# Fused product with its rounded parts first, a re-ordered start, two sums of a double tile started later, and the last output and its stores in another order

## The chip, the cores and the metric

The kernel runs on one core of one Trainium2 chip. The metric is the time of one execution in device microseconds, lower is better. A core has five engines that run side by side, each with its own instruction stream: PE (matrix products, into the eight banks of PSUM), DVE (elementwise work of vectors), ACT (activations and copies), POOL (a further, slower elementwise engine) and SP, which here only issues transfers. They wait for each other by semaphores.

## The reference

Three layers follow each other on 4608 tokens (8 batches of 576) with 512 features. All data are fp32.

```python
def _attn_ref(q, k, v, p):                 # 8 batches, 8 heads, 576 x 64; p: 32 packed rows
    p_packed = sm_attn(p, k, v)
    return sm_attn(q, p_packed, p_packed)

def _moe_ref(x, w_gate, w_val, w_out, rms_g):       # 512 -> 1536 -> 512
    rms = np.sqrt(np.mean(x * x, axis=-1, keepdims=True) + 1e-06)
    xn = x / rms * rms_g
    g = xn @ w_gate
    silu = g * (1.0 / (1.0 + np.exp(-g)))
    return silu * (xn @ w_val) @ w_out

def _moe2_ref(x, w1, w2, w3, w_out):                # 512 -> 1024 -> 1024 -> 512
    h = (x @ w1) * (x @ w2) @ w3
    return h @ w_out
```

## The kernel before

**Three products for one.** PE multiplies fp32 numbers quickly in a rounded format. Every operand is split into a rounded part `hi` (a copy on ACT) and the rest `lo` (a subtraction on DVE that needs `hi`); a product is `hi·hi + hi·lo + lo·hi`, three matmuls added in PSUM. A matmul of 512 columns starts about 0.227 us behind the one in front of it.

**Stage 1, the start.** Since nothing stands between `w3` and the last `w_out`, their product `wf` (1024 x 512) is formed once. `fuse(half, c, rows)` on PE does chunk c of 8 for half of `wf`: four blocks (`rows`) of three matmuls each. Before it, SP loads the chunk (`load_fuse`), ACT rounds (`fuse_split`), DVE subtracts. Into this work the attention of batch 0 is woven by hand, as *items*: S1 (scores), AT (transposes), PV, PT, G, S2, Z, SS (sum of squares), M (gate and value weights folded with the packed values, six pieces). An item has its PE part and behind it parts on ACT and DVE; two items that use the same banks need the older one's parts done (`xy_free`). The order of the calls is written out once for each engine, and `FIRST_ITEMS` numbers the items. From SS comes the reciprocal root of the mean square: `ms` on DVE, `eps` added and the power taken on POOL (`inverse_rms`), a store and a broadcast load through memory (`spread_r`), POOL scales `a2T` with it (`scale_a2`), ACT and DVE split it (`a2_split`); the loop needs that.

**Stage 2, the loop.** 192 slots n (`into` and `outof` on PE) go over the gated layer of all batches; the next batch's items lie between them (`SLOT_ITEMS`). Gate and value have one bank each, so `into(n)` waits until DVE has read slot n-1 (`u_ready`, `h_ready`). `wo_split` splits the output weights in slots of the first batch.

**Stage 3, the last layer.** A tile of 256 columns (t = 0) and four *double tiles* of 512 go through four pairs p each; g counts the 20 groups. A group has seven products in a Strassen-like scheme, P1, P6, P7, P4, P5, P2, P3, which DVE adds up (`e1`, `u2`, `u3`, `c21`, ...) into `h` (four quarters, each a product of two sums), which is split again and goes through `outof2` or `outof_wide` with `wf`. The first double tile starts at g = 4. Its operands are sums of quarters of x that POOL makes in `sum_x(t)`: `b12`, `t2`, then `t4` (for P4) and `t1` (for P5); ACT and DVE split each. Between P6 and P7 of g = 4 PE does `outof2(3)`; P7 then needs the banks that DVE empties in `evict2`.

**The end.** The last group's `outof_wide` (16 blocks of three matmuls: 8 column blocks m, each for f = 1 and f = 0) is followed by DVE's `add_out(m)` and a store of block m.

## Time and profile before

| what | value |
|---|---|
| time of three runs | median 1333.63 us (1332.37 to 1334.44) |
| the profiled execution: own time, span of its instructions | 1333.3 us, 1331.5 us |
| PE busy | 1314.6 us, 99% of the span, 8592 matmuls |
| DVE, ACT, POOL busy | 875.4, 411.1, 125.2 us |
| PE's granted clock, mean | 0.998 of full speed |

The span goes from the first to the last instruction; the execution's own time lies 1.8 us above it. A matmul's end is modelled and overlaps the next one's start, so PE counts as busy up to 0.16 us after it could have started the next; a share of 99% leaves room for short waits that the busy time does not show. They are seen in the starts: where two matmuls of 512 columns lie further apart than 0.227 us, PE stood.

### The profile page before, as it was taken

Reading aid. Unit: us, or ns where it says so; the run is one execution under the profiler, and the core shown is the slowest. Engines: PE = TensorE matmul, PEld = TensorE weight load, DVE = VectorE, ACT = ScalarE, POOL = GpSimd, SP = SyncE. Lnnn points to the kernel's source line nnn. Section 1 sums busy time; section 2 is a strip of 40 time slices with the busy share of each in tenths; the row PEclk is TensorE's granted clock in tenths of the full one; section 3 lists DMA queues with packets and bytes.
Section 4 is the critical chain, followed back from the end, with each engine's and each line's share of the span. In section 5 each row is a group of like instructions: output and inputs, shape, how many; then the busy total and the mean of one; then the engine's idle time right before and its main releaser. Section 6 shows DMA issues by size and latency. Waiting matters only on the chain.

```text
span 1331.5 us, 21676 instructions
## 1 busy us (share of the span) xinstructions
PE 1314.6 (99%) x8592; PEld 1090.7 (82%) x8592; DVE 875.4 (66%) x1363; ACT 411.1 (31%) x785; POOL 125.2 (9%) x101
## 2 busy tenths in 40 slices
PE   8999999999999999999999999899999999999998
PEld 6788888888878788887889899788888888888886
DVE  4668657576565765756754667766776686677665
ACT  5344433434434344343333433210200120112000
POOL 0200101001000010010100531100200010020000
PEclk9999999999999999999999999999999999999999
DMA  9683434343534435333326486745454335545202
GB/s 352 223 282 124 156 124 154 126 163 109 176 97 162 160 117 162 122 118 105 113 74 231 184 313 261 245 136 182 141 175 158 127 119 197 175 144 192 91 1 64
DMA packets 117203, 211.41 MB, mean 159 GB/s; under 512 B 33904, under 2 KB 35952, under 8 KB 114032
## 3 DMA queue, kind: packets, MB, share of 16 engines
q1 hardware_dynamic: 90992, 203.73, 44.8%
q10 hardware_dynamic: 26112, 6.30, 2.1%
q8 instruction: 69, 1.13, 0.4%
q14 instruction: 30, 0.25, 0.1%
HBM read 168.04 MB, written 41.96 MB: 158 GB/s over the span
## 4 chain that ended last, share of the span: by engine, by line
PE 96%; DVE 2%; DMA 1%; issue 1%; ACT 0%; SPq 0%; DVEq 0%; ACTq 0%
PE psum L946 9%; PE psum L948 8%; PE psum L947 8%; PE psum L834 8%; PE psum L836 8%; PE psum L835 8%; PE psum L860 7%; PE psum L859 7%; PE psum L858 7%; PE psum L988 4%; PE psum L990 4%; PE psum L989 4%; PE psum L793 3%; PE psum L777 1%; PE psum L874 1%; PE psum L872 1%
## 5 line engine op out<-in xcount | busy, mean ns | idle before, releaser
L834 PE MATMUL psum<-a_hi,m_hi 128*128 128x288 f32 x768 | 235.5, 307 | 1.9 <-DVE g_s L1529 1.0
L836 PE MATMUL psum<-a_hi,m_lo 128*128 128x288 f32 x768 | 226.3, 295 | 0.0
L835 PE MATMUL psum<-a_lo,m_hi 128*128 128x288 f32 x768 | 226.3, 295 | 0.0
L834 PEld LDWEIGHTS psum<-a_hi,m_hi 128*128 128x128 f32 x768 | 144.2, 188 | 47.5 <-issue 39.3
L1529 DVE SCALAR_TENSOR_TENSOR g_s<-g_s,psum 128x288 f32<-128x288 f32 x192 | 86.7, 452 | 129.6 <-ACT g_s L1243 128.7
L860 PE MATMUL psum<-g_hx,wo_lo 128*128 128x512 f32 x384 | 152.1, 396 | 0.0
L859 PE MATMUL psum<-g_hx,wo_hi 128*128 128x512 f32 x384 | 151.4, 394 | 0.0
L1248 ACT CAST g_hx<-g_h 128x288 fp32r<-128x288 f32 x192 | 83.1, 433 | 219.5 <-DVE g_h L1535 214.5
L858 PE MATMUL psum<-g_hx,wo_hi 128*128 128x512 f32 x384 | 150.2, 391 | 0.0
L835 PEld LDWEIGHTS psum<-a_lo,m_hi 128*128 128x128 f32 x768 | 144.4, 188 | 5.1
L836 PEld LDWEIGHTS psum<-a_hi,m_lo 128*128 128x128 f32 x768 | 144.1, 188 | 0.0
L1547 DVE TENSOR_TENSOR g_hx<-g_h,g_hx 128x288 fp32r<-128x288 f32 x192 | 90.4, 471 | 70.1 <-ACT g_hx L1248 70.1
L1307 ACT CAST hhd<-hd_raw 128x1024 fp32r<-128x1024 f32 x16 | 16.9, 1054 | 317.7 <-DVE hd_raw L1633 309.0
L1243 ACT ACTIVATE g_s<-psum 128x288 f32<-128x288 f32 x192 | 78.9, 411 | 91.3 <-PE psum L836 89.9
L988 PE MATMUL psum<-wf_hi,hhd 128*128 128x512 f32 x256 | 100.4, 392 | 0.1
L990 PE MATMUL psum<-wf_hi,hd_lo 128*128 128x512 f32 x256 | 99.7, 389 | 0.0
L989 PE MATMUL psum<-wf_lo,hhd 128*128 128x512 f32 x256 | 99.7, 389 | 0.0
L946 PE MATMUL psum<-xd_hi,w_hi 128*128 128x512 f32 x224 | 88.0, 393 | 4.7 <-DVE u L1654 4.7
L1476 DVE TENSOR_TENSOR bd<-bd,psum 128x512 f32<-128x512 f32 x96 | 65.9, 687 | 40.6 <-PE psum L990 39.5
L1535 DVE SCALAR_TENSOR_TENSOR g_h<-g_s,psum 128x288 f32<-128x288 f32 x192 | 87.1, 454 | 6.9 <-DVE g_s L1529 0.3
L947 PE MATMUL psum<-xd_lo,w_hi 128*128 128x512 f32 x224 | 87.8, 392 | 0.0
L948 PE MATMUL psum<-xd_hi,w_lo 128*128 128x512 f32 x224 | 87.6, 391 | 0.0
(188 smaller groups left out, 2437.6 us busy)
## 6 DMA issues: line engine op xcount, KB each, us to landing
w_in<-in_w_gate SPq DMA_DIRECT2D x24, 1024.0 KB, 7.3
w_in<-in_w_val SPq DMA_DIRECT2D x24, 1024.0 KB, 5.2
wb_hi<-w_scratch SPq DMA_DIRECT2D x56, 256.0 KB, 2.8
wb_lo<-w_scratch SPq DMA_DIRECT2D x56, 256.0 KB, 3.1
w_hi<-w_scratch SPq DMA_DIRECT2D x49, 256.0 KB, 2.9
w_lo<-w_scratch SPq DMA_DIRECT2D x49, 256.0 KB, 3.7
kT<-in_kT SPq DMA_DIRECT2D x8, 1152.0 KB, 7.5
v_sb<-in_v SPq DMA_DIRECT2D x8, 1152.0 KB, 10.1
```

Source lines behind the costliest of these rows:

```text
L834: nc.tensor.matmul(in_ps[which], hi, a2_hi[:, t, par, :], start=par == 0, stop=False)
L835: nc.tensor.matmul(in_ps[which], hi, a2_lo[:, t, par, :], start=False, stop=False)
L836: last = nc.tensor.matmul(in_ps[which], lo, a2_hi[:, t, par, :], start=False, stop=par == 1)
L858: nc.tensor.matmul(out_ps[m], hi, hh, start=f == 0, stop=False)
L859: nc.tensor.matmul(out_ps[m], hi, hl, start=False, stop=False)
L860: last = nc.tensor.matmul(out_ps[m], lo, hh, start=False, stop=f == FC - 1)
L946: nc.tensor.matmul(dst, hi, xhi[:, c, :], start=c == 0, stop=False)
L947: nc.tensor.matmul(dst, hi, xlo[:, c, :], start=False, stop=False)
L948: last = nc.tensor.matmul(dst, lo, xhi[:, c, :], start=False, stop=c == 1)
L988: nc.tensor.matmul(dst, hhd[:, f, cols], wf_hi[:, chunk, :], start=f == 1, stop=False)
L989: nc.tensor.matmul(dst, hhd[:, f, cols], wf_lo[:, chunk, :], start=False, stop=False)
L990: last = nc.tensor.matmul(dst, hld[:, f, cols], wf_hi[:, chunk, :], start=False, stop=f == 0)
```

## The change

Six things, in the order of the program:

1. `fuse` issues the four `hi·hi` matmuls of a chunk first, then the four `hi·lo`, then the four `lo·hi`, and waits for each part only there; the last chunk keeps the order of before, block by block. Seven warming matmuls are issued and not eight.
2. The third chunk is loaded ahead of `kT`. The order of items and chunks is written anew on PE, ACT and DVE; the two rounding steps (`exp1(1, 0)`, `a2_split`) of the loop's first needs stand ahead of `wf_evict(1)`. The item M(0, 2) moves from the start into slot 0 of the loop, its DVE part to the end of slot 1, and `wo_split(0)` into slot 1.
3. `eps` is added on DVE and no longer on POOL; `spread_r(0)` is issued ahead of `load_w_in(0, 2)`.
4. For the first double tile POOL starts `t4` and `t1` only when the fourth group's last quarter of `h` is there (`h12_ready`), and DVE makes `lo` of the first half of `h` ahead of the `lo` of P6's operand.
5. In the last `outof_wide`, f = 0 of block m follows f = 1 of block m+3 (`LEAD`), where all of f = 1 came first.
6. The last two column groups of x change places, so that the blocks m = 0..3 hold the batches' remainders; of each of their two stores one is issued by SP and one by ACT.

```diff
-FIRST_ITEMS = [..., ("Z", 0, 0), ("Z", 0, 1), ("M", 0, 0), ("SS", 0, 0), ("S1", 1, 0), ("M", 0, 1), ("S1", 1, 1), ("M", 0, 2)]
+FIRST_ITEMS = [..., ("Z", 0, 0), ("Z", 0, 1), ("SS", 0, 0), ("M", 0, 0), ("S1", 1, 0), ("M", 0, 1), ("S1", 1, 1)]
-WARM = 8
+WARM = 7
 # SP
-            load_fuse(0, 0)
-            load_fuse(0, 1)
+            for c in range(3):
+                load_fuse(0, c)
             load_kp(0)
...
             store_wf(0)
+            spread_r(0)
             load_w_in(0, 2)
-            spread_r(0)
...
-                    sp.dma_start(out_batches[B - 1, P * m:P * (m + 1), :], bd[:, m, :]).then_inc(out_stored, 16)
+                    sp.dma_start(out_batches[2 * m, TILE2:S, :], bd[0:REST, m, :]).then_inc(out_stored, 16)
                 else:
-                    for h in range(2):
-                        sp.dma_start(out_batches[2 * (m - 4) + h, TILE2:S, :], bd[REST * h:REST * (h + 1), m, :]).then_inc(out_stored, 16)
+                    sp.dma_start(out_batches[B - 1, P * (m - 4):P * (m - 3), :], bd[:, m, :]).then_inc(out_stored, 16)
 # POOL
                 pool.wait_ge(x_sum_ready, 4 * t + 2)
+                if t == 1:
+
+                    pool.wait_ge(h12_ready, PAIRS)
 # PE, fuse
+                for group in ([(m,) for m in rows] if last_chunk else [rows]):
+                    for m in group:
...
+                        nc.tensor.matmul(psum[:, fuse_bank[r], :], w3_hi[half][:, c, P * m:P * (m + 1)], wout_hi[:, c, :],
+                                         start=c == 0, stop=False)
+                    if half == 0 and not last_chunk:
+                        pe.wait_ge(wout_lo_ready, c + 1)
...
+                    if not last_chunk:
+                        pe.wait_ge(w3_lo_ready, FC2 * half + c + 1)
 # PE, the end
-            for f in (1, 0):
-                for m in range(BLOCKS2):
-                    if f == 1:
-                        block_free(GROUPS - 1, m)
-                    outof_wide(GROUPS - 1, m, f)
+            for m in range(BLOCKS2 + LEAD):
+                if m < BLOCKS2:
+                    block_free(GROUPS - 1, m)
+                    outof_wide(GROUPS - 1, m, 1)
+                if m >= LEAD:
+                    outof_wide(GROUPS - 1, m - LEAD, 0)
 # ACT, the end
+            for m in range(4):
+                act.wait_ge(bd_ready, BLOCKS2 * (PAIRS * WIDE - 1) + m + 1)
+                nc.scalar.dma_start(out_batches[2 * m + 1, TILE2:S, :], bd[REST:P, m, :]).then_inc(out_stored, 16)
 # DVE
+                    nc.vector.tensor_scalar(ms[:], ms[:], EPS_RMS, None, ALU.add).then_inc(ms_ready, 1)
...
+                if g < GROUPS - 1:
+                    rest2(1)
                 for u in late[2]:
                     unit(u)
-                if g < GROUPS - 1:
-                    rest2(1)
```

**The first chunk on PE.** Rows of PE's order behind the warming matmuls, first of the kernel before (the lines 809, 810, 811 are the three products of a block):

```order
L996 MATMUL psum<-ident 128x128 x8
L809 MATMUL psum<-wout_hi,w3a_hi 128x512
L810 MATMUL psum<-wout_lo,w3a_hi 128x512
L811 MATMUL psum<-wout_hi,w3a_lo 128x512
L809 MATMUL psum<-wout_hi,w3a_hi 128x512
L810 MATMUL psum<-wout_lo,w3a_hi 128x512
L811 MATMUL psum<-wout_hi,w3a_lo 128x512
```

and of the changed kernel, where a row with x4 stands for the four blocks:

```order
L1015 MATMUL psum<-ident 128x128 x7
L819 MATMUL psum<-wout_hi,w3a_hi 128x512 x4
L824 MATMUL psum<-wout_lo,w3a_hi 128x512 x4
L829 MATMUL psum<-wout_hi,w3a_lo 128x512 x4
L819 MATMUL psum<-wout_hi,w3a_hi 128x512 x4
L824 MATMUL psum<-wout_lo,w3a_hi 128x512 x4
L829 MATMUL psum<-wout_hi,w3a_lo 128x512 x4
L819 MATMUL psum<-wout_hi,w3a_hi 128x512 x4
L824 MATMUL psum<-wout_lo,w3a_hi 128x512 x4
L829 MATMUL psum<-wout_hi,w3a_lo 128x512 x4
L737 MATMUL psum<-kT,pT 32x288 x16
```

The part that needs only the two rounded operands now stands four matmuls ahead of the first that needs `wout_lo`, and eight ahead of the first that needs `w3a_lo`; three chunks stand ahead of the first item (S1, L737).

**The step to the double tile.** DVE's order of the fourth group's end and of the first double tile, before (`h_lo` is the rest of a half of `h`, `xd_lo` that of an operand of the double tile):

```order
L1640 TENSOR_TENSOR e<-e,psum 128x512
L1647 TENSOR_TENSOR h_raw<-e 128x256
L1451 TENSOR_TENSOR xd_lo<-t,xd_hi 128x1024
L1574 TENSOR_TENSOR h_lo<-h_raw,hh 128x512
L1654 TENSOR_TENSOR u<-u,psum 128x512
L1656 TENSOR_TENSOR h_raw<-u 128x256
L1574 TENSOR_TENSOR h_lo<-h_raw,hh 128x512
L1451 TENSOR_TENSOR xd_lo<-xd_raw,xd_hi 128x1024
L1586 TENSOR_TENSOR u2d<-e1d,psum 128x1024
```

and changed:

```order
L1670 TENSOR_TENSOR e<-e,psum 128x512
L1677 TENSOR_TENSOR h_raw<-e 128x256
L1604 TENSOR_TENSOR h_lo<-h_raw,hh 128x512
L1476 TENSOR_TENSOR xd_lo<-t,xd_hi 128x1024
L1684 TENSOR_TENSOR u<-u,psum 128x512
L1686 TENSOR_TENSOR h_raw<-u 128x256
L1604 TENSOR_TENSOR h_lo<-h_raw,hh 128x512
L1476 TENSOR_TENSOR xd_lo<-xd_raw,xd_hi 128x1024
L1616 TENSOR_TENSOR u2d<-e1d,psum 128x1024
```

The `lo` of the first half of `h` has moved ahead of that of P6's operand (`xd_lo<-t`). POOL's rows with their waits there, before and changed:

```order
L692 TENSOR_TENSOR t<-x 128x1024 [waits b11_loaded,x_sum_ready]
L698 TENSOR_TENSOR xd_raw<-x,t 128x1024 [waits prod_done6,b21_loaded,x_sum_ready]
L701 TENSOR_TENSOR xd_raw<-x,t 128x1024 [waits prod_done4]
```

```order
L694 TENSOR_TENSOR t<-x 128x1024 [waits b11_loaded,x_sum_ready]
L703 TENSOR_TENSOR xd_raw<-x,t 128x1024 [waits b21_loaded,prod_done6,h12_ready,x_sum_ready]
L706 TENSOR_TENSOR xd_raw<-x,t 128x1024 [waits prod_done4]
```

The third sum, and the fourth behind it, now wait for `h12_ready`, which DVE gives with the last `h_raw<-u` of the group.

**The end.** PE's order with its waits from block m = 3 on (`hl2_ready0` stands for f = 0), in the changed kernel, where the kernel before had the twelve matmuls of f = 1 for the blocks 4 to 7 in their place:

```order
L1007 MATMUL psum<-wf_hi,hhd 128x512 [waits hl2_ready1,u4_ready]
L1008 MATMUL psum<-wf_lo,hhd 128x512
L1009 MATMUL psum<-wf_hi,hd_lo 128x512
L1007 MATMUL psum<-wf_hi,hhd 128x512 [waits hl2_ready0]
L1008 MATMUL psum<-wf_lo,hhd 128x512
L1009 MATMUL psum<-wf_hi,hd_lo 128x512
L1007 MATMUL psum<-wf_hi,hhd 128x512 [waits hl2_ready1,c11_ready]
L1008 MATMUL psum<-wf_lo,hhd 128x512
L1009 MATMUL psum<-wf_hi,hd_lo 128x512
```

The first block that needs `hl2_ready0` is now the fifth of sixteen and not the ninth. The last stores on SP before:

```order
L614 DMA out<-bd 128x512 [waits bd_ready] x4
L617 DMA out<-bd 64x512 [waits bd_ready]
L617 DMA out<-bd 64x512
L617 DMA out<-bd 64x512 [waits bd_ready]
L617 DMA out<-bd 64x512
```

and changed:

```order
L620 DMA out<-bd 64x512 [waits bd_ready] x4
L622 DMA out<-bd 128x512 [waits bd_ready] x4
L140 UNCONDITIONAL_BRANCH [waits out_stored]
```

SP has eight to issue in the place of twelve, and its last one covers 128 rows; four of 64 rows are issued by ACT.

## Rows read from the trace of the kernel before

**Rows 1.** The page, part 1: busy time, share of the span, count.

```profile
PE 1314.6 (99%) x8592; PEld 1090.7 (82%) x8592; DVE 875.4 (66%) x1363; ACT 411.1 (31%) x785; POOL 125.2 (9%) x101
```

**Rows 2.** The waits of PE, longest first in total: us, times, longest.

```profile
PE psum L946 <- DVE u L1654: 4.7, 1, 4.7
```

**Rows 3.** Timeline of the start: us from the start, duration, what, idle before.

```profile
4.42 0.62 ACT L1126 CAST w3a_hi<-w3a_raw 128x512 fp32r<-128x512 f32 x1 [0.39 <-DMA w3a_raw<-in_w3T]
5.82 0.50 PE L809 MATMUL psum<-wout_hi,w3a_hi 128*128 128x512 f32 x1 [0.79 <-DVE w3a_lo L1409]
```

**Rows 4.** Timeline around the third chunk of the fused product.

```profile
12.66 0.69 DVE L1409 TENSOR_TENSOR w3a_lo<-w3a_raw,w3a_hi 128x512 fp32r<-128x512 f32 x1
...
13.41 0.50 PE L809 MATMUL psum<-wout_hi,w3a_hi 128*128 128x512 f32 x1 [0.65 <-DVE w3a_lo L1409]
```

**Rows 5.** Timeline of PE: three later waits in the fused product.

```profile
32.52 0.50 PE L809 MATMUL psum<-wout_hi,w3a_hi 128*128 128x512 f32 x1 [0.39 <-DVE w3a_lo L1409]
...
35.87 0.50 PE L809 MATMUL psum<-wout_hi,w3b_hi 128*128 128x512 f32 x1 [0.34 <-DVE w3b_lo L1409]
...
42.89 0.50 PE L809 MATMUL psum<-wout_hi,w3b_hi 128*128 128x512 f32 x1 [0.25 <-DVE w3b_lo L1409]
```

**Rows 6.** Timeline of POOL: the reciprocal root of batch 0.

```profile
50.66 1.18 POOL L649 TENSOR_TENSOR ms<-ms,eps_rms 96x6 f32<-96x6 f32 x1 [3.46 <-DVE ms L1337]
51.91 1.34 POOL L653 TENSOR_TENSOR rr<-ms,neg_half 96x6 f32<-96x6 f32 x1
```

**Rows 7.** Timeline of DVE: the rounding rest of batch 0's first half.

```profile
62.05 1.27 DVE L1400 TENSOR_TENSOR a_lo<-a2T,a_hi 128x576 fp32r<-128x576 f32 x1 [0.91 <-ACT a_hi L1119]
```

**Rows 8.** Timeline of PE: slots 1 and 2 of the loop.

```profile
67.78 0.37 PE L834 MATMUL psum<-a_hi,m_hi 128*128 128x288 f32 x1 [0.32 <-DVE g_s L1529]
...
70.28 0.40 PE L834 MATMUL psum<-a_hi,m_hi 128*128 128x288 f32 x1 [0.67 <-DVE g_s L1529]
```

**Rows 9.** Timeline of DVE at the first double tile.

```profile
834.61 2.71 DVE L1451 TENSOR_TENSOR xd_lo<-t,xd_hi 128x1024 fp32r<-128x1024 f32 x1 [0.63 <-ACT xd_hi L1174]
837.24 2.83 DVE L1574 TENSOR_TENSOR h_lo<-h_raw,hh 128x512 fp32r<-128x512 f32 x1
839.99 0.68 DVE L1654 TENSOR_TENSOR u<-u,psum 128x512 f32<-128x512 f32 x1
840.70 0.42 DVE L1656 TENSOR_TENSOR h_raw<-u 128x256 f32<-128x256 f32 x1
...
845.43 1.22 DVE L1586 TENSOR_TENSOR u2d<-e1d,psum 128x1024 f32<-128x1024 f32 x1 [0.48 <-PE psum L948]
...
848.90 1.30 DVE L1458 COPY b_res<-psum 128x512 f32<-128x512 f32 x2 [1.12 <-PE psum L966]
```

**Rows 10.** Timeline of POOL at the first double tile: its two last sums.

```profile
833.56 2.68 POOL L698 TENSOR_TENSOR xd_raw<-x,t 128x1024 f32<-128x1024 f32 x1 [4.56 <-PE psum L948]
836.20 3.32 POOL L701 TENSOR_TENSOR xd_raw<-x,t 128x1024 f32<-128x1024 f32 x1
```

**Rows 11.** Windows there: length, busy by engine, PEclk, DMA share, GB/s.

```profile
836.00:840.80 4.80, 0.13 (x1) 0.02 (x1) 4.77 (x4) 0.00 (x0) 3.52 (x2) 1.00 0.97 318
840.81:844.30 3.49, 3.49 (x8) 2.77 (x9) 1.58 (x3) 3.09 (x4) 0.00 (x0) 0.51 1.04 387
```

**Rows 12.** Timeline of the end: PE, DVE, SP.

```profile
1314.27 0.47 PE L988 MATMUL psum<-wf_hi,hhd 128*128 128x512 f32 x1
...
1317.75 1.23 DVE L1574 TENSOR_TENSOR hd_lo<-hd_raw,hhd 128x1024 fp32r<-128x1024 f32 x1 [1.17 <-ACT hhd L1310]
...
1324.14 5.19 SPq L617 DMA_DIRECT2D out<-bd  x8
```

**Rows 13.** DMA issues: count, KB each, median us to landing.

```profile
r_sb<-r_scratch SPq DMA_DIRECT2D x8, 288.0 KB, 5.0
out<-bd SPq DMA_DIRECT2D x4, 256.0 KB, 2.0
out<-bd SPq DMA_DIRECT2D x8, 128.0 KB, 2.4
```

More of the change, by code:

```diff
@@ L485, in load_x @@
                 loaded = x_loaded if h else (b11_loaded, b21_loaded)[k]
-                sp.dma_start(part, x_halves[2 * t - 1 + h, k]).then_inc(loaded, 16)
+                sp.dma_start(part, x_halves[half_tile(t, h), k]).then_inc(loaded, 16)
             def load_wo(i):
@@ L490, in load_wo @@
                 sp.dma_start(wo_raw[:, rows, :], wo_v[:, rows, :]).then_inc(wo_loaded[i], 16)
-            load_fuse(0, 0)
-            load_fuse(0, 1)
+            for c in range(3):
+                load_fuse(0, c)
             load_kp(0)
-            for c in range(2, 5):
+            for c in range(3, 5):
                 load_fuse(0, c)
@@ L646, in inverse_rms @@
             def inverse_rms(a):
[L647 to L649 removed]
+                pool.wait_ge(neg_ready, 1)
                 pool.wait_ge(ms_ready, a + 1)
@@ L797, in fuse @@
             def fuse(half, c, rows=(0, 1, 2, 3)):
-                pe.wait_ge(w3_lo_ready, FC2 * half + c + 1)
+                last_chunk = c == FC2 - 1
+                pe.wait_ge(w3_hi_ready, FC2 * half + c + 1)
                 if half == 0:
-                    pe.wait_ge(wout_lo_ready, c + 1)
-                for m in rows:
-                    r = 4 * half + m
-                    if c == 0 and r >= 6:
-                        pe.wait_ge(wf_act, r - 5)
-                    cols = slice(P * m, P * (m + 1))
-                    hi, lo, dst = w3_hi[half][:, c, cols], w3_lo[half][:, c, cols], psum[:, fuse_bank[r], :]
-                    nc.tensor.matmul(dst, hi, wout_hi[:, c, :], start=c == 0, stop=False)
-                    nc.tensor.matmul(dst, hi, wout_lo[:, c, :], start=False, stop=False)
-                    last = nc.tensor.matmul(dst, lo, wout_hi[:, c, :], start=False, stop=c == FC2 - 1)
-                    if c == FC2 - 1:
-                        last.then_inc(fuse_done, 1)
+                    pe.wait_ge(wout_hi_ready, c + 1)
@@ new lines, in fuse @@
+                if last_chunk:
+                    pe.wait_ge(w3_lo_ready, FC2 * half + c + 1)
+                    if half == 0:
+                        pe.wait_ge(wout_lo_ready, c + 1)
+                for group in ([(m,) for m in rows] if last_chunk else [rows]):
+                    for m in group:
+                        r = 4 * half + m
+                        if c == 0 and r >= 6:
+                            pe.wait_ge(wf_act, r - 5)
+                        nc.tensor.matmul(psum[:, fuse_bank[r], :], w3_hi[half][:, c, P * m:P * (m + 1)], wout_hi[:, c, :],
+                                         start=c == 0, stop=False)
+                    if half == 0 and not last_chunk:
+                        pe.wait_ge(wout_lo_ready, c + 1)
+                    for m in group:
+                        nc.tensor.matmul(psum[:, fuse_bank[4 * half + m], :], w3_hi[half][:, c, P * m:P * (m + 1)], wout_lo[:, c, :],
+                                         start=False, stop=False)
+                    if not last_chunk:
+                        pe.wait_ge(w3_lo_ready, FC2 * half + c + 1)
+                    for m in group:
+                        last = nc.tensor.matmul(psum[:, fuse_bank[4 * half + m], :], w3_lo[half][:, c, P * m:P * (m + 1)], wout_hi[:, c, :],
+                                                start=False, stop=last_chunk)
+                        if last_chunk:
+                            last.then_inc(fuse_done, 1)
@@ L1235, in _ @@
                     item(*it)
-                if b + 1 < B and s in EXP1:
+                if b + 1 < B and s in EXP1 and n:
                     exp1(b + 1, EXP1.index(s))
@@ L1248, in _ @@
                 nc.scalar.copy(g_hx[f % 2][:, 0, HALF * t:HALF * (t + 1)], g_h[:]).then_inc(hh_ready, 1)
-                if n < SLOTS and t == 0:
+                if 0 < n < SLOTS and t == 0:
                     wo_split(f)
@@ L1481, in _ @@
                 nc.vector.memset(mask[NP * c:NP * (c + 1), NP * c:NP * (c + 1)], 1.0).then_inc(mask_ready, 1)
-            for c in range(3):
+            for c in range(4):
                 fuse_split(0, c)
             shift1(0)
-            fuse_split(0, 3)
+            fuse_split(0, 4)
             sums1(0)
-            fuse_split(0, 4)
-            fuse_split(0, 5)
-            fuse_split(0, 6)
+            for c in range(5, 8):
+                fuse_split(0, c)
+            freed(dve, "G", 0, 0)
             item("S2", 0, 0)
             shift2(0, 0)
+            fuse_split(1, 0)
             inner(0)
-            fuse_split(0, 7)
             sums2(0, 0)
             normalize2(0, 0)
-            fuse_split(1, 0)
             item("S2", 0, 1)
@@ L1548, in _ @@
                                         ALU.subtract).then_inc(hl_ready, 1)
-                if n < SLOTS and t == 0:
+                if n == 1:
+                    item("M", 0, 2)
+                if 0 < n < SLOTS and t == 0:
                     wo_split(f)
```

82 lines of the change are left out of this document (42 added, 40 removed).

## Prediction

> **What bounds the kernel now.** I read the page first: PE is busy for 1314.6 of 1331.5 us [rows 1], and the change takes no matmul away but one that warms. So only time in which PE stands can be won, and what of the end lies behind PE. The waits of PE come next: one is 4.7 us long, at the first double tile, the others are below a microsecond [rows 2]. Then the timelines, at three places.
>
> *The start.* PE begins the fused product at 5.82, when `w3a_lo` is there; the rounded operand was ready at 4.42 + 0.62 = 5.04 [rows 3]. It stands again before the third chunk, with 0.65 us idle shown, whose operands land behind `kT` [rows 4], and three times later with 0.39, 0.34 and 0.25 shown, each for a DVE subtraction [rows 5]. The idle time shown is not the whole loss. A matmul lasts 0.39 in the trace and the next starts 0.227 later, so 0.16 belongs on top; and where a chunk is cut in the middle, its restart (0.50 for 0.39) is 0.11 more.
>
> *The step to the double tile.* PE is through with P1 at 836.0 and P6 starts at 840.8 [rows 11]; it waits for DVE's sum `u` (839.99) [rows 2, 9]. DVE stands before it in two subtractions that take 2.71 and 2.83 us [rows 9], though the same forms take 1.22 (1024 wide; 845.43 shows that length for another add) and under 0.7 alone. POOL's `t4` (833.56, 2.68) and `t1` (836.20, 3.32) run at the same time [rows 10]. The times fit turns: DVE's first subtraction ends 1.08 behind POOL's first sum (837.32 against 836.24), the second 0.55 behind POOL's second (840.07 against 839.52). Alone a POOL sum takes about 2.3: 3.32 less the 1.1 in which DVE finished. The wait has a second price: behind it PE is granted 0.51 of its clock for 3.4 us [rows 11], so P6's twelve matmuls take 4.4 and not 2.8, 1.6 more.
>
> *The end.* SP spends 5.19 us issuing the last eight stores, from 1324.14 to 1329.33, about 0.6 each [rows 12], while the last block is summed by 1326.15. The last store lands 2.3 behind its issue at 1328.74, at 1331.1. Stores of 256 KB land 2.0 behind theirs [rows 13].
>
> **The change, part by part.**
>
> *Start.* What goes: 5.82 to 5.1 is 0.7; 0.65 + 0.16 = 0.8 before the third chunk, which is now loaded 1.25 MB earlier; 0.39 + 0.16 = 0.55; 0.34 + 0.27 = 0.6; 0.25 + 0.27 = 0.5; and three waits too short for the view, estimated at 0.2 each. Together 3.8. I followed the new order engine by engine with the durations of the trace: PE meets each `hi` and each `lo` ready, by 0.1 us at the second chunk, and by 0.4 to 2 later. The tight place is SS, which needs both `wsum` pieces: it comes out within 0.1 of PE's arrival. M(0, 2) costs its 1.2 in slot 0 and not in the start, so nothing. In slots 1 and 2 PE waited for `u` (0.32 and 0.67 shown, 1.3 with the overlap) [rows 8]. M(0, 2) covers the first; but ACT now makes `m_hi` (1.0) ahead of slot 1's tanh, and DVE `m_lo` (1.2) ahead of slot 2's sums, so about 0.9 and 0.3 stay: 0.1 gained. The eighth warming matmul is hidden either way: its time lies before 5.0. The chain to slot 0: POOL's `eps` add, 1.18 us, becomes a DVE operation of 0.2 [rows 6], and SS stands ahead of M(0, 0). Before, the rest of `a2` was ready at 62.05 + 1.27 = 63.3 [rows 7] and slot 0 began at 65.7 (67.78 less twelve matmuls of 0.13 and the 0.47 waited). Now SS is about 3 earlier and the chain 1.0 shorter: 59.2, with slot 0 at 65.7 - 3.8 - 1.3 = 60.6. It holds if `r_sb` lands in its 5.0 [rows 13], with 1.4 to spare. The `ms` add in the other seven batches lies beside PE's slots. I take 3.8 less 0.1 for SS: **3.7**. Bounds: 2.7 (two chunks late by the size of the waits seen, 0.5) and 4.6 (slot waits gone too).
>
> *The first double tile.* Without POOL beside it DVE does: `h_lo` at 833.9 to 834.6, `lo` of P6 834.6 to 835.8, `u` (0.68) to 836.5, `h` (0.42) to 836.9. PE starts P6 at 836.6 where it was 840.8, and with its clock up. POOL starts `t4` at 836.95 and ends at 839.3; DVE's next `h_lo`, ready at 837.6, gets its turn then and ends at 839.9; POOL's `t1` ends at 842.2. ACT has rounded `t4` by 840.4, but DVE's `lo` of P4 gets through only behind POOL: 842.2 + 1.1 = 843.3. Then `u2d` (1.22) to 844.5, `lo` of P5 to 845.6, and `evict2` (two copies, 1.30) [rows 9] to 846.9. P7 waits for `evict2`. PE has done P6 and `outof2(3)` at 836.6 + 2.8 + 5.4 = 844.8 and stands 2.1. Before, P7 started at 850.7 (24 matmuls behind 845.2), with `evict2` done at 850.2. So P7 comes 3.8 earlier, 0.1 of it lost in the restart: **3.7**. What is late next is thus P7. Bounds: 5.9 if POOL and DVE don't take turns there, and 2.3 if POOL's sums take 3.32 each and DVE is pushed back accordingly.
>
> The Trainium skill has the turn-taking too (GPSIMD Engine Reference, Key points: the two share their SBUF interfaces, with contention where DVE has two SBUF inputs). By that rule `u2d` and the copies, which read PSUM, run free, as I have put them; if it held for them too, `t1` would still be over by then, and the sum stays.
>
> *The end.* In the last group f = 1 of the first four blocks runs from 1314.27 for 12 x 0.227 + 0.1, to 1317.1. The fifth block-part now is f = 0 of block 0, and it needs DVE's `hd_lo`, ready at 1317.75 + 1.23 = 1318.98 [rows 12]; before, PE had work until 1319.8. So PE stands from 1317.1 to 1319.1 and ends 2.1 later: a loss of 2.1. Then DVE's last sum ends at 1328.3, SP issues one store at once, which lands after 2.0: 1330.35 where it was 1331.08. The stores gain 2.8, together **0.7**. Bounds: 2.8 if PE did not wait, and a loss of 2.1 if the stores gain nothing.
>
> The Trainium skill speaks against a gain from sharing the issues (DMA: Bandwidth & Descriptors, Issuing engines are not separate DMA queues: a second issuer saves only the issuing time, usually small beside the transfer). By it the end would lose 2.1 and the time be 1328.0; the row decides otherwise, since eight issues took 5.19 us and the last sum was over 2.6 before the last issue began.
>
> *Sum.* 3.7 + 3.7 + 0.7 = 8.1. The profiled execution took 1333.3 (span 1331.5 and 1.8 around it), 0.3 below the median of the runs: **1325.2 us**.
>
> **The rivals.**
>
> *P7 does not wait.* If POOL's sums and DVE's subtractions overlap, the middle gives 5.9: 1323.0. For it: the sums are only 2.4 long in themselves. Against it: both long subtractions end behind a POOL sum [rows 9, 10]. 12%.
>
> *The clock falls in a new gap.* After 4.7 us without a matmul it fell to 1.2 GHz and cost 1.6 [rows 11]; after the 0.67 in slot 2 it stayed up. The new gaps (2.1 at P7, 2.0 at the end) lie between. One fall gives 1326.8, two 1328.4. [...] 12%.
>
> *The start gives half.* Six places of the new order have under 0.5 us to spare; if four cost 0.5 each, the start gives 1.7: 1327.2. 11%.
>
> *The change moves the waits only.* Start 1, middle 0.7 (P7 late and the clock down), end 0: 1331.6, no change to tell. 5%.
>
> *Slower.* Slot 0 waits for the scaled `a2`. `r_sb` now has the 1 MB of `w_in(0, 2)` right behind it in the same queue, and at 51 us `w_in(0, 3)`. If it landed 9.5 us later than its 5.0, slot 0 would start past 69 and all 8.1 be gone; beyond that the kernel is slower, at 12 later 1335.8. Against it: in the trace of before a transfer of 1 MB was issued 0.4 behind it too, and it landed in 5.1. 4%.
>
> **How the numbers follow.** The forecast, with each of the three terms near its size (1323.8 to 1326.8), has 56%. Its point is the prediction. The range takes in P7 without a wait at its lower end and one or two falls of the clock or a half start at its upper end: 1321.9 to 1328.4, with some 12% left out. A measurement here tells 0.2%, 2.7 us, from no change. Faster by more holds in all cases but the last two and a part of the half start with a fallen clock: 0.91; same 0.05; slower 0.04.
>
> **What the changed profile would show.** Right: the first fused matmul at 5.1; the third chunk follows the second with no gap; slot 0 starts at 60 to 61.5; P6 of the first double tile waits about 0.6, and P7 about 2, for `evict2`; DVE's `lo` of P4 is over 2 us long; PE's clock is at 2.4 GHz there; in the last group one wait of about 1.9 for `hd_lo`; the last store lands 2.0 behind its issue. Wrong: a wait for `a2`'s rest before slot 0, for `wsum` before SS, or new waits at P4 and P5.

## The result, and the profile after

| what | before | changed |
|---|---|---|
| median, lowest, highest of five runs each (us) | 1333.55, 1332.37, 1334.44 | 1325.23, 1323.90, 1327.67 |
| ratio of the times, 95% interval | | 0.9941 [0.9926, 0.9955] |
| the profiled execution: own time, span | 1333.3, 1331.5 | 1326.28, 1324.7 |

The change makes the kernel 0.59% faster by the ratio, 8.3 us by the medians; the forecast was 1325.2. The agreement to 0.03 us is luck: the two profiled executions lie 7.0 apart and not the 8.1 of the forecast's sum, and the changed kernel's five runs spread over 3.8 us. One execution of `whole_stores_lead3`, below, took 1451.83 us at a mean granted clock of 0.847, where its other three took 1340.65 to 1342.94; it is left out of every figure. The page after the change, part 1:

```profile
PE 1313.4 (99%) x8590; PEld 1090.2 (82%) x8590; DVE 874.1 (66%) x1371; ACT 410.9 (31%) x785; POOL 121.6 (9%) x92
```

PE's busy time fell by 1.2 us against [rows 1]; the other 5.6 of the 6.8 us of span are time in which PE stood. The waits of PE now:

```profile
PE psum L965 <- DVE b_res L1483: 1.9, 1, 1.9
PE psum L1007 <- DVE hd_lo L1604: 1.8, 1, 1.8
...
PE psum L853 <- DVE g_s L1553: 0.8, 2, 0.4
PE psum L965 <- DVE u L1684: 0.5, 1, 0.5
PE psum L819 <- ACT w3a_hi L1144: 0.4, 1, 0.4
```

The 4.7 of [rows 2] has become 0.5 (`u`, ahead of P6), and two waits of nearly 2 us are new: `b_res` is `evict2`, ahead of P7, and `hd_lo` is the fifth block-part of the last group. Where the time went can be followed by the starts of the same matmul in both traces:

| the same matmul | before | changed | difference | forecast |
|---|---|---|---|---|
| first of the fused product | 5.82 | 5.37 | -0.45 | -0.7 |
| first of slot 0 | 65.72 | 62.68 | -3.04 | -5.1 (M(0, 2) now lies in the slot) |
| first of slot 4 | 76.70 | 74.61 | -2.09 | -3.7 |
| first of stage 3's double tiles (P1, g = 4) | 833.22 | 830.66 | -2.56 | -3.7 |
| first of P7, g = 4 | 850.67 | 844.36 | -6.31 | -7.4 |
| first of the last group's `outof_wide` | 1314.27 | 1308.00 | -6.26 | -7.4 |
| last matmul | 1325.04 | 1320.83 | -4.21 | -5.3 |
| last landing | 1331.08 | 1324.11 | -6.97 | -8.1 |

*Start.* Timeline of PE at the first chunk and at slot 2, changed kernel:

```profile
5.37 2.07 PE L819 MATMUL psum<-wout_hi,w3a_hi 128*128 128x512 f32 x4 [0.45 <-ACT w3a_hi L1144]
7.24 1.12 PE L824 MATMUL psum<-wout_lo,w3a_hi 128*128 128x512 f32 x3
...
67.67 0.40 PE L853 MATMUL psum<-a_hi,m_hi 128*128 128x288 f32 x1 [0.43 <-DVE g_s L1553]
```

PE now starts with ACT's rounded operand, and no wait for a subtraction is left in the fused product. But the matmuls of the first chunk stand 0.427 apart from 5.96 to 7.67, where all others stand 0.227 apart: PE runs at the lower of its two clocks, 1.2 GHz, though the page's PEclk says full speed there. That it is the clock is read from the step: where a trace does grant 0.50, as in warm8 below, the same matmuls stand 0.427 apart too. Six steps take 2.60 us (5.37 to 7.97) and not 1.47, so 1.1 us is lost. In the trace of before the first chunk runs at full speed. So the rule that PE stood wherever two such starts lie more than 0.227 us apart holds only at full clock.

*First double tile.* Timelines of DVE and POOL, changed kernel:

```profile
832.05 1.23 DVE L1476 TENSOR_TENSOR xd_lo<-t,xd_hi 128x1024 fp32r<-128x1024 f32 x1
833.19 0.68 DVE L1684 TENSOR_TENSOR u<-u,psum 128x512 f32<-128x512 f32 x1
...
835.07 2.34 DVE L1604 TENSOR_TENSOR h_lo<-h_raw,hh 128x512 fp32r<-128x512 f32 x1 [0.74 <-ACT hh L1300]
838.06 2.69 DVE L1476 TENSOR_TENSOR xd_lo<-xd_raw,xd_hi 128x1024 fp32r<-128x1024 f32 x1 [0.65 <-ACT xd_hi L1192]
840.67 1.21 DVE L1616 TENSOR_TENSOR u2d<-e1d,psum 128x1024 f32<-128x1024 f32 x1
841.80 1.21 DVE L1476 TENSOR_TENSOR xd_lo<-xd_raw,xd_hi 128x1024 fp32r<-128x1024 f32 x1
842.94 1.28 DVE L1483 COPY b_res<-psum 128x512 f32<-128x512 f32 x2
...
834.46 2.40 POOL L703 TENSOR_TENSOR xd_raw<-x,t 128x1024 f32<-128x1024 f32 x1 [8.14 <-DVE h_raw L1686]
836.82 2.85 POOL L706 TENSOR_TENSOR xd_raw<-x,t 128x1024 f32<-128x1024 f32 x1
```

The `lo` of P6's operand takes 1.23 without POOL beside it (2.71 in [rows 9]), and `u` starts 6.8 us earlier, 2.6 of them from the start. The collision has not gone but moved: the next `h_lo` (2.34) and the `lo` of P4 (2.69) now lie beside POOL's sums, and end 0.55 and 1.08 behind them, to the hundredth as before. It is the same in the traces of before, of the changed kernel and of eleven of the experiments: a subtraction of 512 columns ends 0.55 behind the POOL sum that it meets, one of 1024 columns 1.08 or 1.09. It is not a matter of subtractions, nor of this place: where a later double tile begins, one of the products that form `h` takes 1.83 beside a POOL sum, and ends 0.55 behind it, three times in the trace of before and three in this one; it takes 0.69 alone, and no wait of PE shows there. Timeline of the changed kernel at the second double tile:

```profile
940.13 2.40 POOL L703 TENSOR_TENSOR xd_raw<-x,xd_raw 128x1024 f32<-128x1024 f32 x1 [11.07 <-PE psum L967]
...
941.25 1.83 DVE L1656 TENSOR_TENSOR hd_raw<-c21d 128x512 f32<-128x512 f32 x1
```

In DVE's row above `evict2` comes last, at 842.94 to 844.22, and PE waits for it:

```profile
842.04 0.39 PE L985 MATMUL psum<-wf_hi,h_lo 128*128 128x512 f32 x1
844.36 0.47 PE L965 MATMUL psum<-xd_hi,w_hi 128*128 128x512 f32 x1 [1.93 <-DVE b_res L1483]
```

*The end.* Timeline of PE, then the DMA issues from 1313 us on:

```profile
1310.60 0.39 PE L1009 MATMUL psum<-wf_hi,hd_lo 128*128 128x512 f32 x1
1312.76 0.50 PE L1007 MATMUL psum<-wf_hi,hhd 128*128 128x512 f32 x1 [1.77 <-DVE hd_lo L1604]
```

```profile
out<-bd SPq DMA_DIRECT2D x4, 256.0 KB, 2.2
out<-bd SPq DMA_DIRECT2D x4, 128.0 KB, 2.3
out<-bd ACTq DMA_DIRECT2D x4, 128.0 KB, 2.6
```

PE stands, and every store lands 2.1 to 2.7 behind its issue, the last one 2.14 behind 1321.97, right after DVE's last sum.

### The profile page after: what moved, and what is told of

Same layout as the page of the kernel before. It is cut to its first block, busy times and chain, and to the rows that moved or that the text cites. A ratio compares the mean times of both kernels' runs of the same rounds, so it can differ in the third digit from the quotient of the medians.

```text
span 1324.7 us, 21669 instructions
## 1 busy us (share of the span) xinstructions
PE 1313.4 (99%) x8590; PEld 1090.2 (82%) x8590; DVE 874.1 (66%) x1371; ACT 410.9 (31%) x785; POOL 121.6 (9%) x92
## 4 chain that ended last, share of the span: by engine, by line
PE 95%; DMA 1%; DVE 1%; issue 1%; ACT 1%; POOL 0%; SPq 0%; DVEq 0%; ACTq 0%; POOLq 0%
PE psum L965 8%; PE psum L967 8%; PE psum L966 8%; PE psum L853 8%; PE psum L855 7%; PE psum L854 7%; PE psum L879 7%; PE psum L878 7%; PE psum L877 7%; PE psum L1007 4%; PE psum L1009 4%; PE psum L1008 4%; PE psum L798 3%; PE psum L819 1%; PE psum L782 1%; PE psum L824 1%
```

## The experiments

All are edits of the changed kernel, or of an edit of it. Each was timed beside the kernel before on its own chip (before: 1333.29, 1333.61 and 1333.58 in the three sets).

| kernel | median (range), runs | ratio to before, 95% |
|---|---|---|
| warm8 | 1325.87 (1323.71 to 1326.99), 5 | 0.9939 [0.9925, 0.9952] |
| all_f1_first | 1325.16 (1324.17 to 1326.23), 5 | 0.9937 [0.9924, 0.9949] |
| pool_no_wait | 1328.85 (1328.51 to 1331.62), 5 | 0.9969 [0.9957, 0.9981] |
| p7_early | 1322.72 (1322.50 to 1323.82), 5 | 0.9920 [0.9907, 0.9932] |
| by_block_fuse | 1326.68 (1326.29 to 1327.22), 4 | 0.9947 [0.9934, 0.9961] |
| dve_order_back | 1326.97 (1325.99 to 1327.72), 4 | 0.9948 [0.9932, 0.9965] |
| halves_from_sp | 1327.22 (1326.00 to 1327.92), 4 | 0.9952 [0.9937, 0.9966] |
| p7_early_lead6 | 1322.61 (1321.69 to 1322.72), 4 | 0.9916 [0.9902, 0.9931] |
| p7_early_f1_first | 1322.59 (1321.33 to 1323.29), 4 | 0.9917 [0.9902, 0.9932] |
| whole_stores_f1_first | 1343.41 (1341.92 to 1343.80), 5 | 1.0074 [1.0060, 1.0088] |
| whole_stores_lead3 | 1340.65, 1341.01, 1342.94 | 1.0059 [1.0043, 1.0074] |
| best_of_all | 1340.59 (1339.51 to 1340.75), 5 | 1.0050 [1.0037, 1.0063] |

### warm8: is it the missing warming matmul?

```diff
-WARM = 7
+WARM = 8
```

> The changed kernel with eight warming matmuls again in the place of seven. In the changed kernel's trace the first fused matmuls start 0.43 us apart from 5.37 to 7.67 and 0.227 only behind that, where in the kernel before they were 0.23 apart from the first; the clock is low there for 2.6 us, which costs 1.2. Theory: the missing warming matmul leaves PE idle longest just where the clock would rise, so with eight the spacing is 0.227 from the first fused matmul on and the time is 1.2 lower than the changed kernel's (about 1324.0 by its median of 1325.2, 1325.1 in the profiled execution). Rival: when the clock rises in the first microseconds varies from execution to execution whatever PE does; then this kernel's runs spread over 3 to 4 us as the changed kernel's do (1323.9 to 1327.7) and its median is the same within 0.5. Second rival: the warming matmuls now end after the rounded operand is there and delay the first fused one, 0.1 to 0.4 later.

Its trace has the first chunk at full speed; timeline of PE:

```profile
4.91 1.19 PE L819 MATMUL psum<-wout_hi,w3a_hi 128*128 128x512 f32 x4
5.94 0.85 PE L824 MATMUL psum<-wout_lo,w3a_hi 128*128 128x512 f32 x3
```

That looked like the theory, and slot 4 starts at 72.69, 4.01 ahead of before, more than the 3.7 forecast. The median says otherwise (1325.87, not lower), and so do the other traces. Of nine read with seven warming matmuls seven have a slow stretch in the first chunk (0.6 to 2.7 us long) and two have none; of three with eight, two have one. The first rival fits: when the clock rises in the first 8 us varies between executions, whatever of the two numbers is used. The second rival (0.1 to 0.4 later) is not seen: the first fused matmul is at 4.9 to 5.1.

This trace showed another thing, at the end, behind the wait for `hd_lo`. Timeline of PE, then windows ahead of the slow stretch, in it and behind it (length, busy by engine, PEclk, DMA share, GB/s):

```profile
1312.74 0.63 PE L1008 MATMUL psum<-wf_lo,hhd 128*128 128x512 f32 x1
1313.17 0.63 PE L1009 MATMUL psum<-wf_hi,hd_lo 128*128 128x512 f32 x1
...
1310.67:1312.30 1.63, 1.62 (x6) 1.31 (x7) 0.61 (x1) 0.00 (x0) 0.00 (x0) 0.92 0.00 0
1312.30:1315.30 3.00, 3.00 (x8) 2.31 (x7) 0.76 (x2) 0.00 (x0) 0.00 (x0) 0.50 0.33 87
1315.30:1318.00 2.70, 2.70 (x13) 2.25 (x12) 1.28 (x2) 0.00 (x0) 0.00 (x0) 0.97 0.41 109
```

The granted clock is 0.50 for 3.4 us, from some 1.4 us after the end of the wait of 1.94 on, and the last matmul comes 14.46 us behind the group's first in the place of 12.83: 1.6 lost. This is the rival "the clock falls in a new gap", in one execution.

### pool_no_wait and dve_order_back: what carries the double tile's 3.7 us?

```diff
 # pool_no_wait
-                if t == 1:
-                    pool.wait_ge(h12_ready, PAIRS)
 # dve_order_back
-                if g < GROUPS - 1:
-                    rest2(1)
                 for u in late[2]:
                     unit(u)
+                if g < GROUPS - 1:
+                    rest2(1)
```

> The changed kernel without POOL's wait for h12_ready ahead of t4; DVE's new order (the lo of h first) stays. Theory: the gain at the first double tile comes from keeping POOL's two sums away from DVE's two subtractions, which else take turns; without the wait POOL's sums run from about 831 to 837 again, both subtractions take 2.3 to 2.8 us, P6 starts some 3.5 us later than in the changed kernel and with the clock low: 1329 to 1330.5. Rival: the order on DVE is what matters, since h_lo finishes ahead of POOL's start; then one subtraction alone is slowed and 1.5 is lost: about 1326.7. Second rival: POOL's earlier sums let P7 start earlier (its wait of 2.1 us goes), and nothing is lost: 1325.2.

> The changed kernel with DVE's order of before at the first double tile (lo of P6's operand, then h_lo), POOL's wait for h12_ready kept. Theory: with POOL out of the way h_lo takes 0.68, so P6 starts 0.7 later (its wait 1.3 in the place of 0.6), POOL's sums start 0.7 later, evict2 with them, and P7 too: 0.7 more, 1325.9, and POOL's wait carries 3 of the 3.7 us. Rival: the order alone matters as much as the wait (pool_no_wait lost 3.6), and 2 or more are lost here.

Without POOL's wait, timelines of DVE and POOL:

```profile
830.21 2.89 DVE L1601 TENSOR_TENSOR h_lo<-h_raw,hh 128x512 fp32r<-128x512 f32 x1
833.03 3.36 DVE L1473 TENSOR_TENSOR xd_lo<-t,xd_hi 128x1024 fp32r<-128x1024 f32 x1
836.31 0.67 DVE L1681 TENSOR_TENSOR u<-u,psum 128x512 f32<-128x512 f32 x1
...
829.88 2.68 POOL L700 TENSOR_TENSOR xd_raw<-x,t 128x1024 f32<-128x1024 f32 x1 [4.84 <-PE psum L964]
832.52 2.78 POOL L703 TENSOR_TENSOR xd_raw<-x,t 128x1024 f32<-128x1024 f32 x1
```

Again each subtraction ends 0.5 and 1.1 behind a POOL sum, PE waits 4.7 us for `u` as in [rows 2], and P6 runs at the low clock (0.427 apart from 837.7 to 840.2). P7 starts 17.40 behind P1 where it is 13.70 in the changed kernel: 3.7 lost, 3.6 by the medians. The main theory holds; the order on DVE does not help when POOL is beside it (17.45 between P1 and P7 in the kernel before, 17.40 here).

With POOL's wait and DVE's old order P6 waits 0.6 longer and P7 comes 0.6 later, as expected. The median lies 1.7 above and not 0.7. In the trace the clock falls behind the wait before P7 (granted 0.50 from 845.5 to 848.9), which costs another 1.6; of the four runs two read a mean clock of 0.999 (1327.72, which is the profiled one, and 1327.47), and two read 1.000 (1325.99 and 1326.48). By the starts of P1 and P7 (14.30 apart here), POOL's wait carries 3.1 of the 3.7 and DVE's order 0.6, and the 0.6 only where POOL waits.

### p7_early: the new wait before P7

```diff
-                if g == PAIRS:
-                    unit(("x", 1, P4))
                 dve.wait_ge(prod_done[P6], g + 1)
...
                 if g == PAIRS:
+                    unit(("x", 1, P4))
+                    evict2()
                     unit(("x", 1, P5))
-                    evict2()
```

> The changed kernel with DVE's order at the first double tile as: u2d, lo of P4, evict2, lo of P5, in the place of lo of P4, u2d, lo of P5, evict2. Theory: P7's wait of 2.1 us is DVE's queue alone, with the two copies of evict2 behind the lo of P5 (1.21 us); brought ahead of it they end by 842.4, and P7 then waits for ACT's second copy (843.05) and starts at 843.1, 1.2 earlier: about 1324.0. Rival: the saved time is given back at P4 or P5, whose lo are then late, or POOL's sums stretch u2d so that nothing is gained: 1325.2.

Timelines of DVE and PE:

```profile
835.56 1.21 DVE L1614 TENSOR_TENSOR u2d<-e1d,psum 128x1024 f32<-128x1024 f32 x1
836.69 2.30 DVE L1476 TENSOR_TENSOR xd_lo<-xd_raw,xd_hi 128x1024 fp32r<-128x1024 f32 x1
838.91 1.28 DVE L1483 COPY b_res<-psum 128x512 f32<-128x512 f32 x2
840.11 1.21 DVE L1476 TENSOR_TENSOR xd_lo<-xd_raw,xd_hi 128x1024 fp32r<-128x1024 f32 x1
...
840.27 0.39 PE L985 MATMUL psum<-wf_hi,h_lo 128*128 128x512 f32 x1
840.51 0.40 PE L965 MATMUL psum<-xd_hi,w_hi 128*128 128x512 f32 x1
```

P7 follows `outof2(3)` with no gap: P1 to P7 takes 11.62 and not 13.70, 2.1 less, and no wait comes up behind it, so neither rival holds. I had expected 1.2, since I let P7 wait for ACT's copies too; it needs only the two banks that DVE empties (`bres_dve`). The median is 2.5 lower and the runs spread over 1.3 us and not 3.8. `u2d`, which reads PSUM, takes its 1.21 with POOL's second sum beside it (835.04 to 837.90); in these traces only DVE operations with two operands in SBUF take turns. This is a better kernel than the changed one: its slowest run, 1323.82, is below the other's fastest.

### all_f1_first, p7_early_lead6, p7_early_f1_first, halves_from_sp: the end

```diff
-LEAD = 3
+LEAD = 7
```

in all_f1_first; p7_early_f1_first has it with p7_early's edit, p7_early_lead6 has LEAD = 6 with it. halves_from_sp, where ACT stores nothing:

```diff
-                    sp.dma_start(out_batches[2 * m, TILE2:S, :], bd[0:REST, m, :]).then_inc(out_stored, 16)
+                    for h in range(2):
+                        sp.dma_start(out_batches[2 * m + h, TILE2:S, :], bd[REST * h:REST * (h + 1), m, :]).then_inc(out_stored, 16)
```

> The changed kernel with LEAD = 7, which in the last outof_wide gives the kernel before's order (all of f = 1, then all of f = 0), the new stores kept. Theory: the new order only makes PE wait for hd_lo (1.94 us in the changed kernel's trace, 1310.6 to 1312.8) and gives nothing back, since DVE's sums (0.69) keep pace with PE (0.68 a block) in either order. Then PE ends 1.9 to 2.1 earlier and so does the kernel: about 1323.2. Rival: with the sums 0.68 apart and not 1.36 for the first four, SP (0.34 to 0.47 an issue) and the shared transfers fall behind, and the last store is issued up to 1.5 later than DVE's last sum, so that 0.5 or less is gained: 1324.7 or more.

> p7_early with LEAD = 6: seven blocks of f = 1 ahead of the first f = 0, so that PE does not wait for hd_lo, but the first two sums are 1.36 apart. Theory: the stores of the first four blocks, two of 64 rows each, need about 1.05 us of the transfers for a block (all_f1_first: DMA busy 0.97 of the time at 319 GB/s), the others 0.68 or less; from the first store on they then need 6.9 us, and only an earlier first store helps. It comes 4.85 us behind the group's first matmul, as with LEAD = 3 (4.76), so the last landing stands 0.1 to 0.4 earlier against the first matmul of the last group than the 16.1 of LEAD = 3, at most 0.1 earlier or later than the 15.7 of LEAD = 7: by the median 1322.3 to 1322.8. Rival: the 2.05 us that PE gains come through, 1320.7.

> p7_early with LEAD = 7, on the same chip as p7_early_lead6. Theory (the stores bound the end): last landing 15.7 behind the first matmul of the last group, as in all_f1_first, and by the median 0.4 less than p7_early's 1322.7: 1322.3. Rival (an execution in which the clock falls after the wait for hd_lo costs p7_early more than its profile shows): the wait is gone, and the runs come out 1 lower with a smaller spread: 1321.7.

> The changed kernel with both half stores of the blocks m = 0..3 issued by SP, none by ACT. Theory: with the sums of these blocks 1.36 apart SP has time for two issues of 0.55 each, so the last store is issued with the last sum and lands at the same time: 1325.2, and the gain of the end came from which blocks are stored in halves, not from the second issuer. Rival: SP falls behind by 0.1 to 0.4 a block, and the last store lands 0.5 to 1.5 later: 1326 to 1326.5.

| first `outof_wide` matmul of the last group to | last matmul | last landing |
|---|---|---|
| changed kernel (LEAD = 3) | 12.83 | 16.11 |
| all_f1_first, p7_early_f1_first (7) | 10.78, 10.75 | 15.68, 15.58 |
| p7_early_lead6 (6) | 10.80 | 15.67 |
| halves_from_sp (3) | 12.85 | 17.08 |

The rival of all_f1_first holds. PE does end 2.05 earlier, but the last landing comes only 0.43 earlier: the stores fall behind. DMA traffic and issues of all_f1_first from 1313 to 1330 us (40 slices of 0.425 us):

```profile
DMA  0000019998999999999961000000000000000000
GB/s 0 0 0 0 0 34 193 284 390 284 284 299 304 342 294 333 395 386 390 390 260 67 5 0 0 0 19 0 0 0 0 0 0 0 0 0 0 0 0 0
...
out<-bd SPq DMA_DIRECT2D x4, 256.0 KB, 3.5
out<-bd SPq DMA_DIRECT2D x4, 128.0 KB, 2.6
out<-bd ACTq DMA_DIRECT2D x4, 128.0 KB, 3.1
```

The transfers are busy throughout: while blocks go out in halves of 64 rows they move mostly 284 to 342 GB/s, with whole blocks 386 to 395. A block is 262 kB, so in halves it takes about 0.87 us and whole 0.68, where DVE makes one each 0.68. The first four blocks so build up a backlog, and every later store lands 3.3 to 3.6 behind its issue. LEAD = 3 spaces the first four sums 1.36 apart, and all stores land in time; that is what its PE wait buys, and it costs as much as it buys. LEAD = 6 and 7 end 0.4 to 0.5 sooner in the traces, and by the medians no difference can be told (1325.16 against 1325.23; 1322.61 and 1322.59 against 1322.72). My estimate for LEAD = 6 held; its 4.85 us is the start of the first f = 0 matmul, and the first store is issued 6.48 behind the group's first matmul with LEAD = 3 and 6 alike. The rival of p7_early_f1_first did not hold.

In halves_from_sp SP keeps step: its last issue is at 1322.63, with DVE's last sum over at 1322.60, as the theory had it. Yet the last store lands 3.09 behind, and the end is 0.97 later. Windows over its stores:

```profile
1318.00:1321.00 3.00, 3.00 (x15) 2.49 (x14) 1.81 (x3) 0.00 (x0) 0.00 (x0) 1.00 0.83 189
1321.00:1324.00 3.00, 0.88 (x4) 0.38 (x2) 1.60 (x3) 0.00 (x0) 0.00 (x0) 1.00 0.97 331
```

So neither expectation is right: the size is the rival's, and SP's issuing is not the cause, since SP is in step; what is late is the transfers. Why halves from one queue leave the transfers later than halves from two is not settled. By the medians this kernel lies 2.0 above the changed one, and the other 1.0 is not explained: its profiled execution has a fallen clock behind the wait for P7 (granted 0.50 from 844.7 to 848.1, 1.6 us), but its other three runs, at 1326.00 to 1327.62, read a mean clock of 1.000. The Trainium skill (DMA: Bandwidth & Descriptors, Issuing engines are not separate DMA queues) gives a second issuer only the time of issuing; here it brought 0.97 us at the landing while SP was in step, once.

### by_block_fuse: what the rounded parts first bring

```diff
-WARM = 7
+WARM = 8
-                for group in ([(m,) for m in rows] if last_chunk else [rows]):
+                for group in [(m,) for m in rows]:
```

> The changed kernel with eight warming matmuls and with fuse block by block again (hi hi, hi lo, lo hi for one block, then the next), all other orders as changed. Theory: the four hi hi products ahead cover DVE's subtractions at the first two chunks; without them the second product of the first block waits for w3a_lo (0.6 to 0.7 later than the first one could start) and the second chunk for its own 0.3 to 0.5; the later chunks have their lo early by the new order of the items. So 1.0 to 1.5 more than warm8: about 1326.8 (1325.9 in warm8's median, which held a fallen clock). Rival: the order of items and loads gives all of the start's gain, and the order within a chunk nothing beyond the first 0.6. Second rival: it carries the whole start, and slot 0 begins 3 or more later than at 61.3.

From the first fused matmul (5.11) to slot 0 (63.40) it takes 58.29 us, against 57.31 in the changed kernel's profile, whose first chunk was as slow; the median is 1.45 above the changed kernel's and 0.8 above warm8's. The waits lie elsewhere than I had put them. At the first chunk no wait shows, presumably since the low clock gave DVE the time. The two that show are in later chunks; timeline of PE:

```profile
38.51 0.40 PE L824 MATMUL psum<-wout_lo,w3b_hi 128*128 128x512 f32 x1
39.08 0.50 PE L829 MATMUL psum<-wout_hi,w3b_lo 128*128 128x512 f32 x1 [0.17 <-DVE w3b_lo L1434]
```

These two steps are 0.57 long in the place of 0.227 (the other at 18.91). So the order within a chunk is worth about 1 us of the start's 2 to 4. The rest is the first rival's, by what is left over: slot 4 still starts 1.6 ahead of before, with a first chunk as slow as the changed kernel's. Which of the loads, the items, the `eps` add and the moved M(0, 2) carries it was not separated.

### Whole stores: whole_stores_f1_first, whole_stores_lead3, best_of_all

```diff
 # SP; ACT stores nothing
-                    sp.dma_start(out_batches[2 * m, TILE2:S, :], bd[0:REST, m, :]).then_inc(out_stored, 16)
+                    sp.dma_start(out_batches[2 * m:2 * m + 2, TILE2:S, :], bd[:, m, :]).then_inc(out_stored, 16)
...
-            sp.wait_ge(out_stored, 16 * (1 + 2 * (WIDE - 1) + 4 + B))
+            sp.wait_ge(out_stored, 16 * (1 + 2 * (WIDE - 1) + 4 + 4))
```

whole_stores_f1_first has LEAD = 7 besides, whole_stores_lead3 WARM = 8, best_of_all LEAD = 7, WARM = 8 and p7_early's order.

> The changed kernel with all of f = 1 first (LEAD = 7) and with each of the blocks m = 0..3 stored by one transfer of 128 rows from SP in the place of two of 64 rows from SP and ACT. In all_f1_first PE ended 2.05 us earlier, but each store landed 3.3 to 3.6 behind its issue in the place of 2.1, and three quarters of it was lost. Theory: what costs is the pairs of half stores, about 0.5 us of the transfers each whatever the rows; 128 rows in one take under 0.68 and keep pace with the sums, so the last lands 2.1 behind its issue and the whole 2.0 are gained: about 1323.2. Rival: 256 KB each 0.68 us is too much for the transfers in any form; then they land 3 or more behind the issue as in all_f1_first, and 1324.5 or more comes out.

> Whole stores as in whole_stores_f1_first, but with the changed kernel's LEAD = 3, and with eight warming matmuls. Theory: PE still stands 1.94 for hd_lo, and the stores were in step already with the sums 1.36 apart, so the form of the stores alone gives nothing: PE's last matmul to the last landing 3.3 us as in the changed kernel, and the time is that of warm8 without a fallen clock at the end (1323.5 to 1324.5). Rival: the clock falls behind the wait of 1.94 us, as it did in warm8's profile (0.427 between matmuls from 1312.3 to 1315.3, 2.2 us lost): 1325.5 to 1326.5.

> Everything that helped in one kernel: eight warming matmuls, evict2 ahead of the lo of P5 and u2d ahead of the lo of P4 on DVE, all of f = 1 first at the end, whole stores. Theory: the terms add, since they lie in different stages: 1325.2 less 0.9 (clock at the start, between 0.5 and 1.3 in the four profiles with seven) less 2.1 (P7) less 2.0 (end) is about 1320.2. Rival: a part of p7_early's gain of 2.5 was one start of its own with a clock that rose early (0.5 lost there in the place of 1.2), and the end's clock did not fall in it; then 1320.8. Above 1321.5 the sum does not hold.

All three are some 15 to 18 us slower than the same kernels without the edit, and it lies behind PE's last matmul in the two traces that show it: in whole_stores_f1_first PE ends at 1317.41 of a span of 1340.3, 22.9 ahead of the end, where it is 5.5 in all_f1_first. Its timeline of SP, and the window of four us in the middle:

```profile
1313.79 9.76 SPq L620 DMA_DIRECT2D out<-bd  x4
1323.59 7.42 SPq L622 DMA_DIRECT2D out<-bd  x4
...
1320.00:1324.00 4.00, 0.00 (x0) 0.00 (x0) 0.00 (x0) 0.00 (x0) 0.00 (x0) 0.83 0.13 51
```

The transfers move 51 GB/s with a share of 0.13, two of 16 engines, and SP takes 9.76 and 7.42 us for four issues each, where it takes 2.51 and 2.92 in all_f1_first. The Trainium skill says why (DMA: Bandwidth & Descriptors, Why a DMA increments its semaphore by 16 and not by 1): the number of engines is the largest up to 16 that divides the outermost sizes of both sides, and on the output's side that size is 2, the two batches. The share of 2/16 agrees. That is an argument from the page and the share; no form with another outermost size was tried. whole_stores_lead3 has no trace that can be read with the others, so for LEAD = 3 only the times show that this form of store costs some 15 us. In best_of_all, 20 us above what was expected, the terms ahead of the stores can be read: P1 to P7 took 11.64, as in p7_early, and PE ended 4.61 ahead of the changed kernel.

## Why the prediction was right, and where not

*The first double tile, 3.7.* Right in size and mechanism: 3.75 between P1's and P7's starts (-2.56 to -6.31), and pool_no_wait takes it back. The turns of DVE and POOL, P6's wait of about 0.6, P7's of about 2 for `evict2`, the `lo` of P4 over 2 us long: all stand in the rows. The rival "P7 does not wait" is out; p7_early shows that what it offered, 2.1, was there to be had by DVE's order.

*The end, 0.7.* Right in its parts: PE lost 2.05 (forecast 2.1), and from the last matmul to the last landing it is 3.28 where it was 6.04, 2.76 gained (2.8). What I didn't see is that the two belong together. Without the wait the stores fall behind, so the bound "2.8 if PE did not wait" could not be reached by a better order of PE alone: all_f1_first gave 1.1 against before.

*The start, 3.7.* This is the term that was mis-sized: 2.1 in the profiled execution, below its bound of 2.7. Of the missing 1.6 the low clock in the first chunk makes 1.1, and the rounded operand came 0.3 later than in the trace of before (5.32 against 5.04); the other traces with the changed `fuse` have the first fused matmul at 4.8 to 5.1, as forecast. The sign "slot 0 starts at 60 to 61.5" was missed, with 62.68. The order itself holds: slot 4 starts 2.1 to 4.0 us ahead of the one trace of before in the eleven traces that have it (median 3.2), with 3.4 to 4.0 in the three where the clock was up from the first fused matmul on. Slots 1 and 2 keep waits of 0.59 and 0.30, for which I had 0.9 and 0.3. The term took the clock of one trace of before, full speed from 5.8 on, as given, and my bounds had no room for it. The Trainium skill has it (TensorE: Matmul & The Clock Gate, Part 1: The HAM clock gate): the number of slow matmuls at a kernel's start differs from run to run. The traces agree, with 0 to 2.7 us of slow stretch.

*Not forecast:* 0.47 between slot 4 and the first double tile. It is within what this stretch varies by: from slot 4 to P1, where the kernels differ in little but the seven `eps` adds, it takes 756.52 in the trace of before and 755.24 to 757.41 in the eleven traces, by short waits of PE that come and go. This variation of 2.2 us is as large as the terms under test, and a single profile cannot tell a gain of a microsecond over the whole span.

*The clock in a new gap* was a rival with 12%, one case or the other. The runs show it as a share of executions instead: of seven traces with the 2 us wait before P7 the clock fell behind it in two, of seven with the wait for `hd_lo` in one, at 1.6 us each, which is the price that was forecast. It does not explain the spread of the changed kernel's runs. Every run's mean clock is on record; the three traces with a fall read 0.999, and of the changed kernel's five runs only the highest, 1327.67, does. The other four read 1.000 and still lie between 1323.90 and 1326.28. The clock of the first chunk, which this mean does not show, and the 2.2 us of the loop can make that much, but what made it in the unprofiled runs is not shown.

*Sum.* Profile against profile 2.1 + 0.5 + 3.75 + 0.7 = 7.0, 1333.3 to 1326.3. The median of five, 1325.2, lies 1.05 below the profiled execution, and before's lay 0.25 above its own; these two make up the missing 1.3 of the medians' 8.3. The forecast's sum was 1.1 too large against the profiles (8.1 for 7.0), a start over-estimated by 1.6 less the 0.47 that nobody forecast, and it met the median by that chance. *Slower by a late `r_sb`* is out: it landed 4.6 behind its issue, at 57.3, and `a2`'s rest was done at 61.9, 0.8 ahead of slot 0.
